# Attention's jobs in the fused tiles in another order, and weight pieces 4 to 7 split by ScalarE and GpSimd

## The reference

```python
# attention (delta rule), per batch b and head h, over 768 steps t
k_n = k / (norm(k) + 1e-6)
y[t]  = q[t] @ state
v_old = state.T @ k_n[t]
state = state + beta[t] * outer(k_n[t], v[t] - v_old)
x = y as (3072, 384)
# moe: softplus between the two products
h = x @ w_in;  g = max(h, 0) + log1p(exp(-abs(h)));  x = g @ w_out
# moe2: h * cos(h) between them
h = x @ w_in2; g = h * cos(h);                       x = g @ w_out2
```

## Time and profile before

| | |
|---|---|
| median of 3 runs | 1063.79 us (1063.72 to 1065.47) |
| the profiled execution | 1073.02 us, span 1071.1 us |
| mean granted TensorE clock | 0.963 |
| lead-in until the first product | 92.3 us |
| tiles 0 to 4 begin at | 92.3, 209.5, 308.5, 406.8, 499.5 us |
| TensorE, VectorE, ScalarE, GpSimd busy | 1004, 736, 500, 325 us |

### The profile page before, as it was taken

How to read it: one execution, slowest core, us unless ns; L and a number is a source line. 1 busy time by engine, 2 the same in 40 slices (tenths; PEclk the granted TensorE clock), 3 DMA queues, 4 the chain that set the end, 5 groups by cost and what they waited for, 6 DMA issues and landing times.

```text
span 1071.1 us, 26065 instructions
## 1 busy us (share of the span) xinstructions
PE 1004.1 (94%) x11416; PEld 857.5 (80%) x11416; DVE 736.0 (69%) x1094; ACT 499.9 (47%) x809; POOL 324.6 (30%) x375
## 2 busy tenths in 40 slices
PE   4588798999999999999999999999999999999997
PEld 4477577778877887787787888899999999999996
DVE  5945768675757656775643697877767777677765
ACT  3434253535354445535444554544545445454443
POOL 2089406940592088039300185200101001010000
PEclk9756899999999999999999999999999999999999
DMA  8032113200310031010000720102002020010101
GB/s 181 18 83 54 45 40 75 51 19 17 62 45 2 17 61 46 12 37 31 16 17 2 236 78 14 57 1 60 1 1 60 1 60 1 1 30 1 30 1 30
DMA packets 100704, 42.66 MB, mean 40 GB/s; under 512 B 76496, under 2 KB 95952, under 8 KB 100592
## 3 DMA queue, kind: packets, MB, share of 16 engines
q1 hardware_dynamic: 96320, 40.12, 14.7%
q10 hardware_dynamic: 4272, 0.89, 0.5%
HBM read 31.56 MB, written 9.44 MB: 38 GB/s over the span
## 4 chain that ended last, share of the span: by engine, by line
PE 80%; DVE 13%; ACT 4%; issue 2%; DMA 0%; SPq 0%; DVEq 0%; ACTq 0%
PE wide L1359 8%; PE wide L1361 8%; PE wide L1360 8%; PE bank L1360 4%; PE bank L1361 4%; PE bank L1359 4%; PE wide L1379 3%; PE wide L1381 3%; PE wide L1380 3%; PE bank L1381 3%; PE bank L1380 3%; PE bank L1379 3%; PE wide L1384 3%; PE wide L1383 3%; PE wide L1385 3%; PE bank L1059 2%
## 5 line engine op out<-in xcount | busy, mean ns | idle before, releaser
L1359 PE MATMUL wide<-x_hi,wi_hi 128*128 128x512 f32 x408 | 168.5, 413 | 1.4 <-DVE x_lo L823 1.4
L1019 DVE TENSOR_TENSOR g_lo<-tmp,g_hi 128x512 fp32r<-128x512 f32 x192 | 163.4, 851 | 6.6
L1361 PE MATMUL wide<-x_hi,wi_lo 128*128 128x512 f32 x408 | 163.8, 402 | 0.0
L1360 PE MATMUL wide<-x_lo,wi_hi 128*128 128x512 f32 x408 | 163.5, 401 | 0.0
L703 ACT ACTIVATE tmp<-wide 128x512 f32<-128x512 f32 x88 | 52.6, 598 | 178.1 <-PE wide L1361 177.8
L1010 DVE SCALAR_TENSOR_TENSOR tmp<-wide,tmp 128x512 f32<-128x512 f32 x88 | 60.4, 687 | 95.5 <-ACT tmp L707 95.5
L1017 DVE CAST g_hi<-tmp 128x512 fp32r<-128x512 f32 x192 | 104.9, 546 | 20.2 <-DVE tmp L1010 0.9
L439 POOL TENSOR_TENSOR inv<-inv,blk 128x31 f32<-128x31 f32 (+15 forms) x155 | 112.6, 726 | 12.1
L457 POOL TENSOR_TENSOR x_lo<-x_raw,x_hi 128x1536 fp32r<-128x1536 f32 x6 | 23.5, 3910 | 271.5 <-ACT x_hi L490 271.5
L1000 DVE TENSOR_SCALAR tmp<-tmp 128x512 f32<-128x512 f32 x96 | 55.0, 573 | 67.9 <-ACT tmp L694 67.9
L436 POOL TENSOR_TENSOR blk<-blk,inv 128x31 f32<-128x31 f32 (+15 forms) x155 | 93.8, 605 | 12.4
(11 more groups left out here) (137 smaller groups left out, 2198.2 us busy)
## 6 DMA issues: line engine op xcount, KB each, us to landing
stage<-in_moe_w_in SPq DMA_DIRECT2D x32, 192.0 KB, 3.4
stage<-in_moe_w_out SPq DMA_DIRECT2D x8, 768.0 KB, 5.9
qn<-in_q SPq DMA_DIRECT2D x24, 192.0 KB, 3.7
res_v<-in_v SPq DMA_DIRECT2D x24, 192.0 KB, 3.6
x_t<-x_res SPq DMA_DIRECT2D x6, 768.0 KB, 3.8
x_raw<-x_t SPq DMA_DIRECT2D x6, 768.0 KB, 5.7
out_x<-res SPq DMA_DIRECT2D x24, 192.0 KB, 3.1
kn<-in_k SPq DMA_DIRECT2D x40, 96.0 KB, 3.0
```

Of the source, the lines that this page charges most:

```text
L1019: nc.vector.tensor_tensor(lo, g, hi.bitcast(FP32), ALU.subtract).then_inc(g_ready, 1)
L1359: mm(dst, wi_hi[:, ft, kt, :], hi[:, kt, :], start=(kt == 0), stop=False)
L1360: mm(dst, wi_hi[:, ft, kt, :], lo[:, kt, :], start=False, stop=False)
L1361: last = mm(dst, wi_lo[:, ft, kt, :], hi[:, kt, :], start=False, stop=(kt == KT - 1))
```

## The change

PE's slots, before and after, for chunks 2 to 5 (T and S jobs only where there is a next chunk; Q0 and P0 at the end of a tile are those of the next chunk). Chunk 1 keeps slots 0 to 6 as they were before, and follows the new order from there.

| slot | before | after | slot | before | after |
|---|---|---|---|---|---|
| 0 | KS0 | KS0 | 18 | KS1 | Y0 |
| 1 | Q0 | - | 19 | Y0 | V1 |
| 3 | P0 | T1 | 20 | V1 | - |
| 5 | T1 | S1 | 21 | Q1 | YT0 |
| 6 | S1 | - | 22 | SN1 | SN1 |
| 8 | - | M1 | 23 | P1 | Q1 |
| 9 | M1 | - | 24 | YT0 | P1 |
| 10, 11 | -, T0 | T0, F1 | 25 | Y1 | Y1 |
| 12, 13 | F1, - | -, V0 | 27 | YT1 | YT1 |
| 14, 15 | V0, S0 | S0, SN0 | 29 | - | Q0 |
| 16, 17 | SN0, - | -, KS1 | 31 | - | P0 |

On VectorE `factors` goes from slot 3 to 1, `take_s` of S1 from 7 to 6, `take_inverse` from 8 to 7, `turn_inverse` from 9 to 8, `take_inner` from 10 to 9, `take_blocks` from 17 and 19 to 16 and 18, and `take_p` of the next chunk to 31. On ScalarE the copies of the next Q0 stand in slot 30, behind `root`, and in tile 0 the rounding of pieces 4, 5, 6 and 7 in slots 7, 12, 15 and 17. GpSimd no longer rounds these pieces; it waits for ScalarE and subtracts in four operations of 384 columns in place of one of 1536. SyncE asks for piece 6 ahead of its wait for V0.

```diff
@@ -42,10 +42,11 @@
 
 FRONT = ("T0", "T1", "S0", "S1")
+AHEAD = ("Q0", "P0")
 FIRST = ("Q0", "P0", "T0", "T1", "S1", ("M1", 0), ("M1", 1), ("F1", 0), "V0", ("F1", 1), "SN0", "KS1", "Y0", "V1", "Q1",
          "SN1", "P1", "YT0", "Y1", "YT1")
-ORDER = ("KS0", "Q0", "P0", "T1", "S1", "M1", "T0", "F1", "V0", "S0", "SN0", "KS1", "Y0", "V1", "Q1", "SN1", "P1", "YT0",
-         "Y1", "YT1")
+ORDER = ("KS0", "T1", "S1", "M1", "T0", "F1", "V0", "S0", "SN0", "KS1", "Y0", "V1", "YT0", "SN1", "Q1", "P1", "Y1", "YT1",
+         "Q0", "P0")
 CONTENT = {}
 
...
@@ -61,12 +62,13 @@
     place_contents(1 if _job in FRONT else 0, _job)
 for _c in range(1, NCH):
     for _job in ORDER:
-        if _job not in FRONT:
+        if _job not in FRONT and _job not in AHEAD:
             place_contents(_c, _job)
         elif _c + 1 < NCH:
             place_contents(_c + 1, _job)
-        if (_c, _job) == (1, "Q0"):
-            place_contents(1, "S0")
+        if (_c, _job) == (1, "KS0"):
+            for _own in ("Q0", "S0", "P0"):
+                place_contents(1, _own)
 
 def weight_pieces(w_in, w_out):
...
@@ -355,12 +357,14 @@
                 store_x2(c - 2)
             sp.wait_ge(filled, cid(c, "Q0", 1) + 1)
             load_q(2 * c + 1)
+            if c == 1:
+                sp.wait_ge(w_split, piece_before(STAGE1, 6) + 1)
+                load_piece(STAGE1, stage1, w1_loaded, pieces1, 6)
             sp.wait_ge(filled, cid(c, "V0", 1) + 1)
             load_v(2 * c + 1)
             if c == 1:
-                for n in (6, 7):
-                    sp.wait_ge(w_split, piece_before(STAGE1, n) + 1)
-                    load_piece(STAGE1, stage1, w1_loaded, pieces1, n)
+                sp.wait_ge(w_split, piece_before(STAGE1, 7) + 1)
+                load_piece(STAGE1, stage1, w1_loaded, pieces1, 7)
             if c + 1 < NCH:
                 sp.wait_ge(filled, cid(c, "V1", 1) + 1)
                 load_v(2 * c + 2)
...
@@ -445,6 +449,15 @@
             pool.wait_ge(w_hi_set, n + 1)
             nc.gpsimd.tensor_tensor(lo, staged(STAGE1, stage1, pieces1, n), hi.bitcast(FP32), ALU.subtract).then_inc(w_split, 1)
+        def low_quarters(n):
+
+            hi, lo = halves(pieces1, n)
+            for i in range(WCH):
+                part = slice(i * DM, i * DM + DM)
+                last = nc.gpsimd.tensor_tensor(lo[:, part], staged(STAGE1, stage1, pieces1, n)[:, part], hi[:, part].bitcast(FP32),
+                                               ALU.subtract)
+            last.then_inc(w_split, 1)
+
         def split(stages, stage, loaded, pieces, n, done):
             hi, lo = halves(pieces, n)
             pool.wait_ge(loaded[stages[n]], loads_until(stages, pieces, n))
...
@@ -466,7 +479,8 @@
         substitute(1)
         pool.wait_ge(w_split, EARLY)
         for n in range(EARLY, NP):
-            split(STAGE1, stage1, w1_loaded, pieces1, n, n - EARLY)
+            pool.wait_ge(w_hi_set, n + 1)
+            low_quarters(n)
         for c in range(2, NCH):
             clean(c)
             scale_blocks(c)
...
@@ -477,7 +491,7 @@
                 pool.wait_ge(h_ready, end)
             else:
                 pool.wait_ge(g_used, end)
-            split(STAGE2, stage2, w2_loaded, pieces2, n, NP - EARLY + n)
+            split(STAGE2, stage2, w2_loaded, pieces2, n, n)
             if n == 2:
                 low_x(TILES)
         for t in range(TILES + 1, 2 * TILES):
...
@@ -632,39 +646,45 @@
             yield
             if c == 1:
                 root(2)
-            take_transposes(c, "Q0", qT)
+                take_transposes(1, "Q0", qT)
             yield
             if c == 1:
                 take_upper(1, 0, "S0")
             yield
-            yield
-            yield
-            if after:
+            if 1 < c < NCH - 1:
                 take_transposes(c + 1, "T1", knT[:, fill_of(c + 1, 1)])
             yield
             yield
+            if c == 1:
+                take_transposes(2, "T1", knT[:, fill_of(2, 1)])
+            yield
+            yield
+            if c == 1:
+                high_weights(4)
             yield
             yield
             fill_diagonal(c, 1)
-            yield
             yield
             if after:
                 take_transposes(c + 1, "T0", knT[:, fill_of(c + 1, 0)])
+            yield
             fill_diagonal(c, 0)
-            yield
             take_outer(c, 0)
             take_outer(c, 1)
             yield
-            yield
-            yield
-            yield
-            yield
-            yield
+            if c == 1:
+                high_weights(5)
+            yield
+            yield
+            yield
+            if c == 1:
+                high_weights(6)
+            yield
+            yield
+            if c == 1:
+                high_weights(7)
             yield
             take_y(c, "Y0")
-            yield
-            yield
-            take_transposes(c, "Q1", qT)
             yield
             yield
             yield
...
@@ -685,6 +709,8 @@
             yield
             if c + 2 < NCH:
                 root(c + 2)
+            if after:
+                take_transposes(c + 1, "Q0", qT)
             yield
             yield
...
@@ -1273,21 +1304,26 @@
             after = c + 1 < NCH
             keys_on_state(c, 0, "KS0")
             yield
-            pe.wait_ge(q_loaded, 64 * c + 32)
-            transposes(c, "Q0", qn)
+            if c == 1:
+                pe.wait_ge(q_loaded, 64 + 32)
+                transposes(1, "Q0", qn)
             yield
             if c == 1:
                 gram(1, 0)
             yield
-            scores(c, 0)
-            yield
-            yield
-            if after:
+            if c == 1:
+                scores(1, 0)
+            elif after:
                 keys_transposed(c + 1, 1)
             yield
-            if after:
+            yield
+            if c == 1:
+                keys_transposed(2, 1)
+            elif after:
                 gram(c + 1, 1)
             yield
+            if c == 1:
+                gram(2, 1)
             yield
             yield
             merge_inner(c, 0)
...
@@ -1315,23 +1351,29 @@
             yield
             solve_values(c, 1, "V1")
             yield
+            yield
+            turn_out(c, "YT0", "Y0")
+            yield
+            add_to_state(c, 1, "SN1")
+            yield
             pe.wait_ge(q_loaded, 64 * c + 64)
             transposes(c, "Q1", qn)
             yield
-            add_to_state(c, 1, "SN1")
-            yield
             scores(c, 1)
             yield
-            turn_out(c, "YT0", "Y0")
-            yield
             read_out(c, 1, "Y1")
             yield
             yield
             turn_out(c, "YT1", "Y1")
             yield
             yield
-            yield
-            yield
+            if after:
+                pe.wait_ge(q_loaded, 64 * c + 96)
+                transposes(c + 1, "Q0", qn)
+            yield
+            yield
+            if after:
+                scores(c + 1, 0)
             yield
         def await_weights(layer, is_in, ft):
```

More of the change, by code:

```diff
@@ L675, in attention @@
             take_x(c, 0, "YT0")
+            yield
+            yield
+            take_transposes(c, "Q1", qT)
+            yield
             yield
@@ L935, in attention @@
             yield
+            if 1 < c < NCH - 1:
+                factors(c + 1)
             yield
@@ L939, in attention @@
             yield
-            if after:
-                factors(c + 1)
+            if c == 1:
+                factors(2)
             yield
-            take_p(c, "P0")
-            yield
+            if c == 1:
+                take_p(1, "P0")
             yield
@@ L979, in attention @@
             yield
+            take_x(c, 0, "YT0")
+            yield
             take_state(c, 1, "SN1")
             yield
+            yield
             take_p(c, "P1")
-            yield
-            take_x(c, 0, "YT0")
             yield
@@ L994, in attention @@
             yield
+            if after:
+                take_p(c + 1, "P0")
             yield
@@ L1281, in attention @@
             yield
-            scores(c, 0)
+            if c == 1:
+                scores(1, 0)
+            elif after:
+                keys_transposed(c + 1, 1)
             yield
             yield
-            if after:
-                keys_transposed(c + 1, 1)
-            yield
-            if after:
+            if c == 1:
+                keys_transposed(2, 1)
+            elif after:
                 gram(c + 1, 1)
             yield
+            if c == 1:
+                gram(2, 1)
             yield
```

## The result

The changed kernel takes 1078.83 us (median of 4, 1076.70 to 1080.34), the kernel before 1063.76 (median of 4): a ratio of 1.0134, 95% interval 1.0101 to 1.0167. It is 15 us slower. I had forecast slower by 3.7 (1067.5 us), with 1074 as the upper end.

The account below looks back on a forecast made before the run. TensorE was busy 1004 of 1071 us, with 23 us of idle time in the five tiles to work on. Idle +4.9, clock -2.7 in tile 0 and +1.5 behind M1: +3.7 on the median 1063.79, 1067.5 us, range 1065 to 1070.

Parts of the forecast that it names:

- Part 2's wait for blk: Ahead of M1: 3.2 us instead of 1.15 in tiles 1 to 4 (+8.2), 2.9 in tile 0 (+1.9).
- Part 3's: Tile ends: P0 waits for ScalarE's copies of Q0, 1.65 us at three ends, 1.1 at the fourth, +6.0 us.
- Part 4's for kn: At T1 in tiles 1 to 3: a wait of about 0.8 us, 2.4 in all as before, so no change.
- x_lo's waits: Since YT0 no longer stands just before Y1, waits of 1.4 us and 0.4 in tile 0 go.
- Part 1: Tile 0, rounding moved to ScalarE: g_lo's 1.7 and kn's 5.2 us of waits go, and 2.7 us of clock cost.
- the clock term behind M1: Products behind M1: a low-clock stretch in tile 3 too, as in the other four tiles, costing +1.5 us.
- rival (a): Slow stretches multiply: 6.8 us behind each of five 3 us waits, 3.4 behind each P0 wait; about 1073 to 1081, chance 0.14.
- M1's half: Behind M1: each of the five 3 us waits brings 6.8 us of low clock, 1.5 more each, +7.5 us.
- Its other half: Behind P0 at tile ends: each wait brings 3.4 us of low clock, +6 us.
- rival (b): Behind M1: the low stretch falls into M1's longer wait, full clock in the products behind; 1060 us, chance 0.17.
- my terms for the order: Idle time in the five tiles from the new slots: mainly waits at M1 (+8.2, +1.9) and P0 (+6.0), less smaller waits removed.

Follow-up runs that it names:

- the weights' part alone: Kernel before in its own order, only the split of pieces 4 to 7 changed (ScalarE rounds, GpSimd subtracts in four parts): 1054.40 us, ratio 0.9907.
- the filled kernel: Changed kernel plus 13 useless 128x512 matmuls on TensorE ahead of merge_inner's wait in each of the five tiles: 1065.99 us.
- The two filled kernels: Useless matmuls ahead of merge_inner's wait: 13 in the changed kernel, 1065.99 us; 4 in the kernel before with the new split of pieces 4 to 7, 1051.27 us.
- the second profile: Kernel before, unchanged, profiled once more: one execution of 1063.91 us, span 1062.0.

## Why the prediction missed

**Right, by its own steps.** Part 2's wait for blk: forecast 3.2 us per tile, and 2.9 in tile 0; found 3.14, and 3.6. Part 3's: forecast 1.65 and 1.1, found 1.38 and 1.0. Part 4's for kn: forecast 0.8, found 0.9 twice and 0.4. x_lo's waits went, but for 0.3 us. Part 1: forecast 6.9+2.7 us; alone it brought 10.1. The sign, and the reason for it (the order costs more than the weights bring), hold.

**The step that failed** is the clock term behind M1. I put it at +1.5 us: one more stretch of 3.4 us, in tile 3, as if a wait of 3.2 us brought the same as one of 1.15. It brought 6.8 us in each of five tiles. Part 1 came as forecast, so the kernel with the weights' part alone is what the order must be held against: 34.1 us of low clock behind M1 against 10.2 there. At 0.375 us for each, the price from the filled kernel, these 23.9 us cost 9.0. The two filled kernels say the same more loosely: 12.8 us less the 3 to 5.5 that the old order pays is 7 to 10. So the term was about +9, and the 7.5 us between it and my 1.5 are two thirds of the 11 us missed.

The rows had it. The wait of 5.2 us for kn with 6.8 us behind it is nearer to 3.2 us than 1.15 is, and rival (a) said so. Its price for M1 was right too: 7.5 us on top of my 1.5 is the 9.0 found. (M1's half alone makes 1067.5+7.5 = 1075.0; the "about 1073" of the prediction is the other half alone.) Its other half did not come: no low clock followed any of the four waits for qT, of 1.0 to 1.4 us. I gave (a) 0.14 and rival (b) 0.17, although my own text called (b) the weaker. And (b), the stretch falling in the wait, was wrong: each stretch began within about a microsecond of M1's start, and only in tile 0 did 0.2 us of it lie in the wait.

**A smaller miss** is in the idle time. From the weights' part alone to the change it grew by 28.8-13.8 = 15.0 us; my terms for the order sum to 11.8. M1's waits were as forecast (+10.2 against +10.1). Tile 0's wait for res_v, gone with the weights' part, was back at 1.4 us, where my terms took 0.5 off; the waits without a releaser grew by 1.0, and those for kn by 0.5. In tile 0 M1 waited 3.6 us and not 2.9, since GpSimd's parts held up two of VectorE's operations ahead of it and not one: beside main(4)'s subtraction also take_inverse's second operation, 1.83 us instead of 1.22. The waits of about 1 us that have no releaser in the profile stay unexplained, before and after.

**The profile I leaned on** was an execution 9 us over the median, with a 5.2 us wait that the second one doesn't have. That part 1's amount held all the same is partly luck: the 6.9 and 2.7 us were read from a wait and a low stretch that are not always there. What GpSimd takes from VectorE turned up in the second profile as other waits, and the weights' part removed those.

## What to carry to other kernels

Moving an operation to an earlier slot helps only if what releases it comes earlier too. Before moving a consumer, find the instruction that releases it and what that one queues behind, and move the release first (one line, 31 us here). Price idle time on the matrix engine with the clock behind it, by the nearest wait in length, and not by the wait that the same instruction had before. A change with two parts is worth running as two: here one part alone was 10 us faster than before and the other 21 us slower.

## What the runs showed of the hardware

An idle time of 3.1 us on TensorE ahead of small matmuls cost 2.6 us more in the clock, nearly as much again; 13 useless matmuls in it gave that back, in every tile. The longer the wait, the longer the low clock behind it, but not strictly. M1's waits of 1.0 to 1.2 us brought 3.4 us of low clock in some tiles and none in others, in each order. M1's wait of 1.5 us in tile 0 brought none in two runs and 6.8 us in a third. One of 2.1 us brought 6.8. Those of 3.1 to 3.6 us brought 6.8 us in all five tiles of the change, while in the run with the scores one tile later one of them brought 3.4 and one 10.2. Waits elsewhere did likewise: res_v's of 1.4 us brought none, of 2.4 us 3.4, of 4.3 us 6.8.

And a VectorE subtraction of 0.69 us took 3.92 beside one GpSimd operation of 3.46 us, and 1.47 beside parts of 1.1.
